# Attention, channel mix and gated convolution on one core: chunk 3's output moved ahead of the scores of chunk 5, two mixes moved up, and loads that wait for an earlier load to land

## The chip, the cores and the metric

The kernel runs on one core of a Trainium2 chip. The metric is the device time of one execution in microseconds. All times come from runs on the chip; the profile is one execution that the hardware profiler recorded.

## What is computed

The input has 2 sequences of 768 positions, 8 heads of 64 features each (512 features in all). Three stages follow one another:

```python
# 1. retention attention with decay lam per head, state kv_state carried along the sequence
intra = (q_b @ k_b.T * Dmask) @ v_b
inter = (q_b * lam_pow) @ kv_state
out[b] = intra + inter
kv_state = lam_block * kv_state + (k_b * rev_pow).T @ v_b
# 2. channel mix with a shift by one position, x = attention output
xk = mu_k * x + (1 - mu_k) * x_prev ; xr = mu_r * x + (1 - mu_r) * x_prev
x2 = sigmoid(xr @ w_r) * (relu(xk @ w_k) ** 2 @ w_v)
# 3. convolution gate of five taps, then projection
y = (sigmoid(conv(x2)) * (x2 @ w_val)) @ w_out
```

All arrays are float32. The reference walks stage 1 in blocks of 64 positions; the kernel uses chunks of 128, which gives the same sums.

## The kernel before

Stage 1 works in 12 chunks of 128 positions, chunks 0 to 5 of the first sequence and 6 to 11 of the second. The first chunk of a sequence has no inter part, the last has no state update. The order of each engine's work is written out by hand, and semaphores tie the engines together.

For a chunk n, **PE** does four things: `scores(n)` (L733, k times q into PSUM), `attend(n)` (L799, the weighted scores times v), `inter(n)` (L783, the state times the decayed q; this is the "state product" of the title) and `update(n)` (L761, decayed k times v). attend and inter add into the same two PSUM banks for a pair of chunks p = n // 2. Each is 8 matmuls in the code, 16 records in the profile. **DVE** weighs the scores with the decay (`weigh`, L508, two instructions of a chunk), makes the next state from the faded old one and the update (`new_state`, L525, L522 for the first of a sequence), and later the second half of the mix (`mix`, L532, four blocks of 128 features; tile xk_f), the low parts that the split products need (`mix_low`, L538, `low`, L543) and the 128x8 operation of L627. **ACT** fades the state (`fade`, L338, four instructions), copies the finished pair of chunks out of PSUM (`evacuate_x`, L330), makes the first half of the mix (`mix_part`, L355) and the high parts (`mix_high`, L361, `high`, L344). **POOL** decays k (`decay_k`, L286) and q (`decay_q`, L298).

What ties them around the change: scores(n) needs the weighing of chunk n - 2. weigh(n) needs scores(n). new_state(n) needs update(n) and the fade of the state before it. inter(n) needs the state of new_state(n - 1) and the decayed q. attend(n) needs the weighing of n. The first mix needs x of chunks 0 to 3, that is evacuate_x(1), which needs attend(3). `STATE_LAST` and `OUT_FIRST` tell which pairs have their inter last or first in the PSUM group.

Stage 2 begins with `hidden(0, 0)` in the middle of the last pair of chunks. It needs the low part of the mixed x (four mix_low) and of the first piece of w_k (`low`, piece 0). From there on PE works through products of 128x512 tiles in three passes each (L717 to L719).

All loads go out from **SP**, in the order in which they are needed: per chunk qk (512 KB) and kv (512 KB; 256 KB for chunks 0, 5 and 11, where k isn't needed), then w_k in four pieces, w_r in two, w_v in four. There are 8 buffers for chunks (`IN_BUFS`): a load of chunk 8 to 11 waits (`free`) until attend and update of the chunk eight before it are done; the others wait for nothing. The w_v loads wait for attend and update of chunk 7, since they lie on chunk buffers.

```python
def free(n):
    if n >= IN_BUFS:
        sp.wait_ge(att_done, n - IN_BUFS + 1)
        sp.wait_ge(update_done, updates(n - IN_BUFS))
```

Of the kernel before, what the change touches and what calls it, by code (L numbers as in the profile page):

```python
# [19 lines left out]
NCH = B * NCB  # L20
T = 512
NT = B * S // T
KT = DM // P
# [6 lines left out]
IN_BUFS = 8  # L30
# [4 lines left out]
CUTS = (0, 384, DM)  # L35
TURNED = 7
OUT_FIRST = 4


LAM_A, LAM_B, MU, CONV = 0, H, H + PAIRS, H + PAIRS + 2 * KT  # L40
# [12 lines left out]
def build(nc, prm_in, qk_in, v0_in, kv_in, w_k, w_v, w_r, w_val, w_out, out):  # L53
    with ExitStack() as ctx:
# [26 lines left out]
        wk_raw = place("wk_raw", [P, KT * DF], wk_at + 16 * KB)  # L81
# [127 lines left out]
        @block.sync  # L209
        def _(sp):  # L210
# [6 lines that stand above are left out]
            def load_qk(n):  # L217
                free(n)
                sp.dma_start(qk[n % IN_BUFS][:, :, :], qk_in[n]).then_inc(qk_here[n % IN_BUFS], 16)

            def load_kv(n):
                free(n)
                first = 0 if has_update(n) else 1
                sp.dma_start(kv[n % IN_BUFS][:, first:, :], kv_in[n, :, first:, :]).then_inc(kv_here[n % IN_BUFS], 16)

            def load_weight(raw, src, i, done):
                sp.dma_start(raw[:, i * PIECE:(i + 1) * PIECE], src[:, i * PIECE:(i + 1) * PIECE]).then_inc(done[i], 16)

            sp.dma_start(prm[:, :], prm_in).then_inc(prm_here, 16)
            load_qk(0)  # L230
            load_qk(1)
            sp.dma_start(kv[0][:, 1, :], v0_in).then_inc(kv_here[0], 16)
            load_qk(2)
            load_kv(1)
            load_qk(3)
            load_kv(2)
            load_qk(4)
            load_kv(3)
            load_qk(5)
            load_kv(4)  # L240
            load_kv(5)
            for p in range(3, NP - 1):
                load_qk(2 * p)
                load_qk(2 * p + 1)
                load_kv(2 * p)
                load_kv(2 * p + 1)
            load_qk(NCH - 2)
            load_qk(NCH - 1)
            load_weight(wk_raw, w_k, 0, wk_here)
            load_kv(NCH - 2)  # L250
            load_kv(NCH - 1)
            for i in range(1, 4):
                load_weight(wk_raw, w_k, i, wk_here)
            for i in range(2):
                load_weight(wr_raw, w_r, i, wr_here)
            sp.wait_ge(att_done, IN_BUFS)
            sp.wait_ge(update_done, updates(IN_BUFS - 1))
            for i in range(4):
                load_weight(wv_raw, w_v, i, wv_here)

            sp.wait_ge(h_done, FT * NT)
            for i in range(4):
                src = w_val if i < 2 else w_out
                sp.dma_start(w2_raw[:, i * PIECE:(i + 1) * PIECE],
                             src[:, i % 2 * PIECE:(i % 2 + 1) * PIECE]).then_inc(w2_here[i], 16)

            for n in range(OUT_CH):
                if n < OUT_CH - 1:
                    sp.wait_ge(out_ready, n + 1)
                    sp.dma_start(out[n * CH:(n + 1) * CH, :], out_sb[n // CT][:, n % CT, :]).then_inc(stored, 16)  # L270
                else:
                    for half in range(2):
                        cols = slice(CUTS[half], CUTS[half + 1])
                        sp.wait_ge(out_ready, n + 1 + half)
                        sp.dma_start(out[n * CH:(n + 1) * CH, cols], out_sb[n // CT][:, n % CT, cols]).then_inc(stored, 16)
            sp.wait_ge(stored, 16 * (OUT_CH + 1))
# [44 lines left out]
        def _(act):  # L321
            def evacuate_x(p):

                b, c = at(2 * p)
                cols = slice(b * SEG + HALO + c * CH, b * SEG + HALO + (c + 2) * CH)
                first = out_banks(2 * p)[0]
                act.wait_ge(att_done, 2 * p + 2)
                if p == OUT_FIRST:
                    act.wait_ge(inter_done, inters(2 * p + 1))
                nc.scalar.copy(x[:, :, cols].rearrange("p (g a) i -> p g a i", g=2),  # L330
                               ps[:, first:first + 2, :].rearrange("p g (a i) -> p g a i", a=2)).then_inc(x_ready, 1)

            def fade(n):

                act.wait_ge(state_ready, updates(n - 1))
                for a in range(PAIRS):
                    cols = slice(a * D, (a + 1) * D)
                    nc.scalar.activation(faded[:, cols], state[:, n % 4, cols], ACT.Copy,  # L338
                                         scale=qdec[:, a, CH - 1:CH]).then_inc(faded_ready, 1)
# [82 lines left out]
            fade(2)  # L422
            fade(3)
            evacuate_x(1)
            fade(4)
            for k in range(KT):
                mix_part(0, k, 0)
            evacuate_x(2)
            fade(7)
            for k in range(3):  # L430
                mix_high(0, k, 0)
            fade(8)
            evacuate_x(3)
            high(wk, wk_raw, 0, wk_here, wk_hi)
            fade(9)
            mix_high(0, 3, 0)
            high(wk, wk_raw, 1, wk_here, wk_hi)
            fade(10)
            for i in range(2, 4):
# [61 lines left out]
        def _(dve):  # L501
# [125 lines left out]
            nc.vector.tensor_scalar(om[:, :], prm[:, MU:MU + 2 * KT], -1.0, 1.0, ALU.mult, ALU.add).then_inc(om_ok, 1)  # L627
            dve.wait_ge(halo_ok, B)
            dve.wait_ge(om_ok, 1)
            for p in range(2, NP):  # L630
                new_state(2 * p)
                if p + 1 < NP:
                    weigh(2 * p + 2)
                    weigh(2 * p + 3)
                new_state(2 * p + 1)
                if p == 2:
                    mix(0, 0, 0)
                    mix(0, 1, 0)
                    mix(0, 2, 0)
                if p == 3:  # L640
                    mix(0, 3, 0)
                    mix_low(0, 0, 0)
                    mix_low(0, 1, 0)
                    mix_low(0, 2, 0)
                if p == 4:
                    mix_low(0, 3, 0)
                    low(wk, wk_raw, 0, wk_hi, wk_lo)
            for i in range(1, 4):
                low(wk, wk_raw, i, wk_hi, wk_lo)
# [63 lines left out]
        def _(pe):  # L713
# [56 lines left out]
            def inter(n):  # L770
                b, c = at(n)
                if c == 0:
                    return
                pe.wait_ge(qd_ready, inters(n))
                pe.wait_ge(state_ready, updates(n - 1))
                if opens(n, True):
                    if n < NCH - 2:
                        pe.wait_ge(x_ready, n // 2)
                    else:
                        pe.wait_ge(p_ready, 2 * n + 2)  # L780
                for a in (0, 2, 1, 3):
                    for row in range(2):
                        last = nc.tensor.matmul(place_of(n, row, a), state[rows_of(row), n % 4, a * D:(a + 1) * D],  # L783
                                                qd[rows_of(row), n % 4, a * P:(a + 1) * P],
                                                start=(opens(n, True) and a % 2 == 0),
                                                stop=(n == 2 * OUT_FIRST + 1 and a % 2 == 1), skip_group_check=True)
                last.then_inc(inter_done, 1)

            def attend(n):
                b, c = at(n)  # L790
                i = n % IN_BUFS
                pe.wait_ge(kv_here[i], 16 * (n // IN_BUFS + 1))
                pe.wait_ge(p_ready, 2 * n + 2)
                if n == 2 * OUT_FIRST:
                    pe.wait_ge(x_ready, OUT_FIRST)
                for a in range(PAIRS):
                    for row in range(2):
                        h = head_of(row, a)
                        last = nc.tensor.matmul(place_of(n, row, a), kv[i][:, 1, h * D:(h + 1) * D],  # L799
                                                pT[:, n % 4, row, a * P:(a + 1) * P],  # L800
                                                start=(opens(n, False) and a % 2 == 0),
                                                stop=(a % 2 == 1 and n % 2 == 1 and n // 2 != OUT_FIRST),
                                                skip_group_check=True)
                last.then_inc(att_done, 1)

# [94 lines left out]
            attend(2)  # L900
            scores(4)
            update(2)
            scores(5)
            update(3)
            inter(3)
            attend(3)
            update(4)
            for p in range(2, NP):
                if p + 1 < NP:
                    scores(2 * p + 2)  # L910
                    scores(2 * p + 3)
                if p == OUT_FIRST:
                    attend(2 * p)
# [86 lines left out]
```

## Time and profile before

| | us |
|---|---|
| median of 3 runs | 276.83 |
| lowest and highest | 275.75, 277.29 |
| the profiled execution | 276.0 |
| its span | 274.2 |
| PE busy | 269.9 |
| DVE busy | 166.0 |
| ACT busy | 125.4 |
| POOL busy | 23.6 |

The granted TensorE clock was 1.00 of full speed over the whole span. The span runs from the first to the last instruction; times in the views count from its start. In a timeline a row gives the start, the time from start to end of the merged instructions, engine and line, the operation, its tiles, the number of records and, in brackets, how long the engine stood idle before it and what ended that. Rows of neighbouring instructions overlap a little, since an instruction's end lies behind the next one's start. So what an instruction costs its engine is the distance from its start to the next one's start.

### The profile page before, as it was taken

The page shows a single profiled execution, that of the slowest core. Times are in us where ns is not written, and L with a number is a line of the kernel's source. Part 1 is how long each engine was busy: PE and PEld are TensorE (multiplying, and loading weights), DVE is VectorE, ACT ScalarE, POOL GpSimd, SP SyncE. Part 2 cuts the span into 40 slices and gives each one's busy share as a digit, 9 for nine tenths or more (in the row PEclk, how much of TensorE's full clock was granted, in tenths as well). Part 3 has the DMA queues.
Part 4 walks back from the last instruction along what each step waited for, and adds up shares of the span by engine and source line. Part 5 has one row for each costly group of instructions (what it writes and reads, how often), then busy time and mean ns, then how long its engine had stood idle before and what let it go on. Part 6 is the DMA issues. An engine that isn't in the chain of part 4 may idle for free.

```text
span 274.2 us, 4270 instructions
## 1 busy us (share of the span) xinstructions
PE 269.9 (98%) x1746; PEld 226.3 (83%) x1746; DVE 166.0 (61%) x258; ACT 125.4 (46%) x223; POOL 23.6 (9%) x25
## 2 busy tenths in 40 slices
PE   8999999999999999999999999999999999999996
PEld 7889977888888888888888888888888888888886
DVE  5866999998581125465885553429969599325000
ACT  2237788977582124365721234748217306412121
POOL 1667750000000000000000000000000000000000
PEclk9999999999999999999999999999999999999999
DMA  7999996000000000000000000530000000310323
GB/s 215 408 410 406 406 407 253 0 0 2 0 0 0 2 0 0 0 2 0 0 0 2 2 0 0 174 134 0 0 0 2 0 0 0 117 38 0 115 82 111
DMA packets 7506, 22.57 MB, mean 82 GB/s; under 512 B 960, under 2 KB 1216, under 8 KB 7488
## 3 DMA queue, kind: packets, MB, share of 16 engines
q1 hardware_dynamic: 7488, 22.31, 21.4%
q8 instruction: 14, 0.23, 0.3%
q14 instruction: 4, 0.03, 0.0%
HBM read 19.16 MB, written 3.15 MB: 81 GB/s over the span
## 4 chain that ended last, share of the span: by engine, by line
PE 96%; DVE 2%; DMA 1%; issue 0%; ACT 0%
PE ps L717 28%; PE ps L719 28%; PE ps L718 28%; PE ps L799 4%; PE ps L733 4%; PE ps L783 2%; PE ps L761 2%; DMA prm<-in_prm 1%; DVE dec L608 1%; DVE pT L508 0%; DVE qdec L589 0%; ACT out_sb L414 0%
## 5 line engine op out<-in xcount | busy, mean ns | idle before, releaser
L717 PE MATMUL ps<-xk_h,wk_h 128*128 128x512 f32 x96 | 37.5, 391 | 0.0
L718 PE MATMUL ps<-xk_l,wk_h 128*128 128x512 f32 x96 | 37.4, 389 | 0.0
L719 PE MATMUL ps<-xk_h,wk_l 128*128 128x512 f32 x96 | 37.4, 389 | 0.0
L717 PE MATMUL ps<-kk_h,wv_h 128*128 128x512 f32 x96 | 37.3, 389 | 0.0
L718 PE MATMUL ps<-kk_l,wv_h 128*128 128x512 f32 x96 | 37.3, 389 | 0.0
L719 PE MATMUL ps<-kk_h,wv_l 128*128 128x512 f32 x96 | 37.3, 389 | 0.0
L571 DVE SCALAR_TENSOR_TENSOR gate<-x,prm,gate 128x512 f32<-128x512 f32 x48 | 32.6, 748 | 0.0
L547 DVE SCALAR_TENSOR_TENSOR kk_f<-ps,ring 128x512 f32<-128x512 f32 x24 | 16.6, 691 | 24.1 <-ACT ring L367 24.1
L384 ACT ACTIVATE gate<-x,prm 128x512 f32<-128x512 f32 x12 | 8.7, 725 | 43.2 <-DVE x L557 43.2
L367 ACT ACTIVATE ring<-ps 128x512 f32<-128x512 f32 x24 | 14.3, 597 | 26.7 <-PE ps L719 26.7
L717 PEld LDWEIGHTS ps<-xk_h,wk_h 128*128 128x128 f32 x96 | 18.0, 188 | 4.0 <-issue 0.3
L719 PEld LDWEIGHTS ps<-xk_h,wk_l 128*128 128x128 f32 x96 | 18.0, 188 | 3.8
L718 PEld LDWEIGHTS ps<-kk_l,wv_h 128*128 128x128 f32 x96 | 18.0, 188 | 3.8
L719 PEld LDWEIGHTS ps<-kk_h,wv_l 128*128 128x128 f32 x96 | 18.0, 188 | 3.8
L557 DVE TENSOR_TENSOR x<-ps,r 128x512 f32<-128x512 f32 x12 | 8.3, 690 | 21.1 <-PE ps L719 21.1
L718 PEld LDWEIGHTS ps<-xk_l,wk_h 128*128 128x128 f32 x96 | 18.0, 188 | 3.7
L717 PEld LDWEIGHTS ps<-kk_h,wv_h 128*128 128x128 f32 x96 | 18.0, 188 | 3.7
L719 PE MATMUL ps<-w_h,gl 128*128 128x512 f32 (+2 forms) x52 | 19.6, 376 | 0.0
L718 PE MATMUL ps<-w_l,gh 128*128 128x512 f32 (+2 forms) x52 | 19.6, 376 | 0.0
L717 PE MATMUL ps<-w_h,gh 128*128 128x512 f32 (+2 forms) x52 | 19.5, 375 | 0.0
L717 PE MATMUL ps<-xr_h,wr_h 128*128 128x512 f32 x48 | 18.7, 389 | 0.0
L718 PE MATMUL ps<-xr_l,wr_h 128*128 128x512 f32 x48 | 18.7, 389 | 0.0
(74 smaller groups left out, 487.5 us busy)
## 6 DMA issues: line engine op xcount, KB each, us to landing
qk<-in_qk SPq DMA_DIRECT2D x12, 512.0 KB, 11.3
kv<-in_kv SPq DMA_DIRECT2D x9, 512.0 KB, 12.8
out<-out_sb SPq DMA_DIRECT2D x11, 256.0 KB, 2.0
wk_raw<-in_w_k SPq DMA_DIRECT2D x4, 512.0 KB, 14.2
wv_raw<-in_w_v SPq DMA_DIRECT2D x4, 512.0 KB, 12.5
wr_raw<-in_w_r SPq DMA_DIRECT2D x2, 512.0 KB, 15.0
w_raw<-in_w_val SPq DMA_DIRECT2D x2, 512.0 KB, 4.4
w_raw<-in_w_out SPq DMA_DIRECT2D x2, 512.0 KB, 6.9
```

The costliest lines, as they stand in the source:

```text
L367: nc.scalar.activation(ring[:, n % 4, :], ps[:, bank_of("mlp", t, n), :], ACT.Relu).then_inc(relu_ready, 1)
L384: nc.scalar.activation(like(t, gate[t][:, k, :]), x_cols(t, k, HALO), ACT.Copy, scale=prm[:, col:col + 1]).then_inc(tap0, 1)
L547: nc.vector.scalar_tensor_tensor(out=kk_f[:, n, :], in0=ps[:, bank_of("mlp", t, n), :], scalar=0.0, in1=ring[:, n % 4, :], op0=ALU.max, op ...
L557: nc.vector.tensor_tensor(x_cols(t, m, 1), like(t, ps[:, bank_of("mlp", t, FT + KT + m), :]), like(t, r[:, m, :]), ALU.mult).then_inc(x2_r ...
L571: nc.vector.scalar_tensor_tensor(out=like(t, gate[t][:, k, :]), in0=x_cols(t, k, HALO - j), scalar=prm[:, col:col + 1], in1=like(t, gate[t ...
L717: nc.tensor.matmul(to, left(0), right(0), start=(i == 0), stop=False)
L718: nc.tensor.matmul(to, left(0), right(1), start=False, stop=False)
L719: done = nc.tensor.matmul(to, left(1), right(0), start=False, stop=(i == last))
L733: last = nc.tensor.matmul(ps_s[n % 2][row][:, cols], qk[i][rows_of(row), 1, cols], qk[i][rows_of(row), 0, cols], start=True, stop=True)
L761: last = nc.tensor.matmul(ps[rows_of(row), ps_u[n % 2], a * D:(a + 1) * D], kdec[:, n % 4, at_k:at_k + D], kv[i][:, 1, h * D:(h + 1) * D], ...
L783: last = nc.tensor.matmul(place_of(n, row, a), state[rows_of(row), n % 4, a * D:(a + 1) * D], qd[rows_of(row), n % 4, a * P:(a + 1) * P], ...
L799: last = nc.tensor.matmul(place_of(n, row, a), kv[i][:, 1, h * D:(h + 1) * D], pT[:, n % 4, row, a * P:(a + 1) * P], start=(opens(n, False ...
```

## The change

On PE, attend(3) and inter(3) go ahead of scores(5), attend first, and update(4) goes between scores(6) and scores(7). For pair 1 the inter part is now the last to add into PSUM, so evacuate_x(1) waits for inter(3) too. On ACT two mix_parts go ahead of fade(4), and mix_high(3) goes up. On DVE mixes 0 and 1 go ahead of new_state(4), mix 3 ahead of the fourth pair's work, mix_low 3 beside the other three. On SP every load from the fifth on waits until an earlier load has landed.

```diff
+STATE_LAST = (1, OUT_FIRST)
...
+            def qk_landed(n):
+
+                sp.wait_ge(qk_here[n % IN_BUFS], 16 * (n // IN_BUFS + 1))
...
             load_qk(2)
+            qk_landed(0)
             load_kv(1)
+            qk_landed(1)
             load_qk(3)
+            kv_landed(0)
             load_kv(2)
+            qk_landed(2)
             load_qk(4)
+            kv_landed(1)
             load_kv(3)
...
             for p in range(3, NP - 1):
+                qk_landed(2 * p - 1)
                 load_qk(2 * p)
+                kv_landed(2 * p - 2)
                 load_qk(2 * p + 1)
+                kv_landed(2 * p - 1)
                 load_kv(2 * p)
+                qk_landed(2 * p)
                 load_kv(2 * p + 1)
+            qk_landed(NCH - 3)
             load_qk(NCH - 2)
+            kv_landed(NCH - 4)
             load_qk(NCH - 1)
+            kv_landed(NCH - 3)
             load_weight(wk_raw, w_k, 0, wk_here)
+            qk_landed(NCH - 2)
             load_kv(NCH - 2)
+            qk_landed(NCH - 1)
             load_kv(NCH - 1)
-            for i in range(1, 4):
-                load_weight(wk_raw, w_k, i, wk_here)
-            for i in range(2):
-                load_weight(wr_raw, w_r, i, wr_here)
+            sp.wait_ge(wk_here[0], 16)
+            load_weight(wk_raw, w_k, 1, wk_here)
+            kv_landed(NCH - 2)
+            load_weight(wk_raw, w_k, 2, wk_here)
+            kv_landed(NCH - 1)
+            load_weight(wk_raw, w_k, 3, wk_here)
+            sp.wait_ge(wk_here[1], 16)
+            load_weight(wr_raw, w_r, 0, wr_here)
+            sp.wait_ge(wk_here[2], 16)
+            load_weight(wr_raw, w_r, 1, wr_here)
...
-                if p == OUT_FIRST:
+                if p in STATE_LAST:
                     act.wait_ge(inter_done, inters(2 * p + 1))
...
             evacuate_x(1)
+            mix_part(0, 0, 0)
+            mix_part(0, 1, 0)
             fade(4)
-            for k in range(KT):
-                mix_part(0, k, 0)
+            mix_part(0, 2, 0)
+            mix_part(0, 3, 0)
             evacuate_x(2)
             fade(7)
-            for k in range(3):
+            for k in range(KT):
                 mix_high(0, k, 0)
...
-            mix_high(0, 3, 0)
...
             dve.wait_ge(om_ok, 1)
+            mix(0, 0, 0)
+            mix(0, 1, 0)
             for p in range(2, NP):
...
                 if p == 2:
-                    mix(0, 0, 0)
-                    mix(0, 1, 0)
                     mix(0, 2, 0)
+                    mix(0, 3, 0)
                 if p == 3:
-                    mix(0, 3, 0)
-                    mix_low(0, 0, 0)
-                    mix_low(0, 1, 0)
-                    mix_low(0, 2, 0)
+                    for k in range(KT):
+                        mix_low(0, k, 0)
                 if p == 4:
-                    mix_low(0, 3, 0)
                     low(wk, wk_raw, 0, wk_hi, wk_lo)
...
             update(2)
+            attend(3)
+            inter(3)
             scores(5)
             update(3)
-            inter(3)
-            attend(3)
-            update(4)
             for p in range(2, NP):
                 if p + 1 < NP:
                     scores(2 * p + 2)
+                    if p == 2:
+                        update(4)
                     scores(2 * p + 3)
```

The two edits of the stop flag in inter and attend follow `STATE_LAST` and are left out here.

PE, around chunks 3 to 7, before. qk_98 to qk_101 are the buffers of chunks 4 to 7, kv_104 to kv_106 those of chunks 2 to 4; L733 is scores, L761 update, L783 inter, L799 attend.

```order
L733 MATMUL ps<-qk_98 128x128 x8
L761 MATMUL ps<-kv_104,kdec 64x64 x8
L733 MATMUL ps<-qk_99 128x128 x8
L761 MATMUL ps<-kv_105,kdec 64x64 x8
L783 MATMUL ps<-qd,state 64x128 x8
L799 MATMUL ps<-pT,kv_105 64x128 x8
L761 MATMUL ps<-kv_106,kdec 64x64 x8
L733 MATMUL ps<-qk_100 128x128 x8
L733 MATMUL ps<-qk_101 128x128 x8
L783 MATMUL ps<-qd,state 64x128 x16
```

The same place now, where the lines of the file have moved: L764 is scores, L792 update, L814 inter, L830 attend.

```order
L764 MATMUL ps<-qk_98 128x128 x8
L792 MATMUL ps<-kv_104,kdec 64x64 x8
L830 MATMUL ps<-pT,kv_105 64x128 x8
L814 MATMUL ps<-qd,state 64x128 x8
L764 MATMUL ps<-qk_99 128x128 x8
L792 MATMUL ps<-kv_105,kdec 64x64 x8
L764 MATMUL ps<-qk_100 128x128 x8
L792 MATMUL ps<-kv_106,kdec 64x64 x8
L764 MATMUL ps<-qk_101 128x128 x8
L814 MATMUL ps<-qd,state 64x128 x16
```

attend(3) and inter(3) moved from behind update(3) to before scores(5), and update(4) moved into the pair of scores(6) and scores(7).

DVE, from the weighing of chunks 3 and 4 on, before. L508 weighs, L525 and L522 make a state, L532 mixes, L538 makes the low part of the mixed x.

```order
L508 TENSOR_TENSOR pT<-ps,dec 128x512 x4
L525 TENSOR_TENSOR state<-faded,ps 128x256
L508 TENSOR_TENSOR pT<-ps,dec 128x512 x2
L525 TENSOR_TENSOR state<-faded,ps 128x256
L627 TENSOR_SCALAR om<-prm 128x8
L525 TENSOR_TENSOR state<-faded,ps 128x256
L508 TENSOR_TENSOR pT<-ps,dec 128x512 x4
L532 SCALAR_TENSOR_TENSOR xk_f<-x,om,xk_f 128x512 x3
L522 COPY state<-ps 128x256
```

The same place now (L541 weighs, L558 and L555 make a state, L565 mixes).

```order
L541 TENSOR_TENSOR pT<-ps,dec 128x512 x4
L558 TENSOR_TENSOR state<-faded,ps 128x256
L541 TENSOR_TENSOR pT<-ps,dec 128x512 x2
L558 TENSOR_TENSOR state<-faded,ps 128x256
L660 TENSOR_SCALAR om<-prm 128x8
L565 SCALAR_TENSOR_TENSOR xk_f<-x,om,xk_f 128x512 x2
L558 TENSOR_TENSOR state<-faded,ps 128x256
L541 TENSOR_TENSOR pT<-ps,dec 128x512 x4
L565 SCALAR_TENSOR_TENSOR xk_f<-x,om,xk_f 128x512 x2
L555 COPY state<-ps 128x256
```

Two of the mixes moved in between the 128x8 operation and new_state(4), which is the third state update of these rows.

## Rows read from the trace of the kernel before

**Rows 1.** The page: span, PE's busy time, GB/s in 40 slices of 6.9 us.
```profile
span 274.2 us, 4270 instructions
...
PE 269.9 (98%) x1746; PEld 226.3 (83%) x1746; DVE 166.0 (61%) x258; ACT 125.4 (46%) x223; POOL 23.6 (9%) x25
...
GB/s 215 408 410 406 406 407 253 0 0 2 0 0 0 2 0 0 0 2 0 0 0 2 2 0 0 174 134 0 0 0 2 0 0 0 117 38 0 115 82 111
```

**Rows 2.** Timeline of PE, 34 to 41 us: attend(8) and the first hidden tile.
```profile
34.63 0.66 PE L799 MATMUL ps<-pT,kv 128*64 128x128 f32 x8
35.89 1.53 PE L799 MATMUL ps<-pT,kv 128*64 128x128 f32 x24 [0.61 <-issue]
...
40.65 0.47 PE L717 MATMUL ps<-xk_h,wk_h 128*128 128x512 f32 x1
```

**Rows 3.** Timeline of DVE, 35 to 42 us: low part of w_k's first piece.
```profile
39.30 1.21 DVE L543 TENSOR_TENSOR wk_l<-wk_raw,wk_h 128x1024 fp32r<-128x1024 f32 x1
```

**Rows 4.** Timeline of PE, 16 to 24 us: update(2) to inter(4) and inter(5).
```profile
16.98 0.69 PE L761 MATMUL ps<-kv,kdec 128*64 128x64 f32 x16
17.59 1.16 PE L733 MATMUL ps<-qk 64*128 64x128 f32 x16
18.68 0.69 PE L761 MATMUL ps<-kv,kdec 128*64 128x64 f32 x16
19.30 0.67 PE L783 MATMUL ps<-qd,state 64*64 64x128 f32 x16
19.89 1.09 PE L799 MATMUL ps<-pT,kv 128*64 128x128 f32 x16
20.82 0.64 PE L761 MATMUL ps<-kv,kdec 128*64 128x64 f32 x16
21.38 2.06 PE L733 MATMUL ps<-qk 64*128 64x128 f32 x32
23.37 1.10 PE L783 MATMUL ps<-qd,state 64*64 64x128 f32 x32
```

**Rows 5.** Instruction packets: all (page), 0 to 33.4 us, 33.4 to 33.6 us.
```profile
q8 instruction: 14, 0.23, 0.3%
...
q8 instruction: 3, 0.05, 0.6%
...
q8 instruction: 1, 0.02, 34.3%
```

**Rows 6.** Busy times by stretch: stretch, length, then busy us (instructions) of each engine.
```profile
0.00:33.40 33.40, 31.99 (x562) 29.00 (x564) 24.77 (x50) 15.32 (x37) 19.26 (x22) 1.00 0.96 368
...
0.00:208.00 208.00, 205.98 (x1456) 172.90 (x1457) 136.67 (x213) 104.88 (x188) 23.55 (x25) 1.00 0.25 93
0.00:236.70 236.70, 234.68 (x1583) 196.65 (x1584) 160.87 (x250) 117.50 (x209) 23.55 (x25) 1.00 0.22 84
```

**Rows 7.** Timelines of POOL and ACT: decay of q 3, evacuate_x(1).
```profile
17.18 1.28 POOL L298 TENSOR_TENSOR qd<-qk,qdec 128x512 f32<-128x512 f32 x1
...
21.04 1.02 ACT L330 COPY x<-ps 128x1024 f32<-128x1024 f32 x1 [1.23 <-PE ps L799]
```

**Rows 8.** Timeline of DVE, 18 to 29 us: states, the 128x8 operation, weighings, mixes.
```profile
18.30 0.41 DVE L525 TENSOR_TENSOR state<-faded,ps 128x256 f32<-128x256 f32 x1
...
20.33 0.70 DVE L627 TENSOR_SCALAR om<-prm 128x8 f32<-128x8 f32 x1
23.14 0.42 DVE L525 TENSOR_TENSOR state<-faded,ps 128x256 f32<-128x256 f32 x1 [2.12 <-ACT faded L338]
23.48 2.48 DVE L508 TENSOR_TENSOR pT<-ps,dec 128x512 f32<-128x512 f32 x4
25.88 2.77 DVE L532 SCALAR_TENSOR_TENSOR xk_f<-x,om,xk_f 128x512 f32<-128x512 f32 x3
```

**Rows 9.** Data packets from 0 to 33.4 us; loads of qk from issue to landing.
```profile
q1 hardware_dynamic: 3682, 12.24, 95.2%
...
DMA to landing us min/median/max: 3.9/11.3/15.7
```

More of the change, by code:

```diff
@@ L227, in load_weight, with kv_landed @@
                 sp.dma_start(raw[:, i * PIECE:(i + 1) * PIECE], src[:, i * PIECE:(i + 1) * PIECE]).then_inc(done[i], 16)
+            def qk_landed(n):
+                sp.wait_ge(qk_here[n % IN_BUFS], 16 * (n // IN_BUFS + 1))
+            def kv_landed(n):
+                sp.wait_ge(kv_here[n % IN_BUFS], 16 * (n // IN_BUFS + 1))
             sp.dma_start(prm[:, :], prm_in).then_inc(prm_here, 16)
@@ L233, in _ @@
             load_qk(2)
+            qk_landed(0)
             load_kv(1)
+            qk_landed(1)
             load_qk(3)
+            kv_landed(0)
             load_kv(2)
+            qk_landed(2)
             load_qk(4)
+            kv_landed(1)
             load_kv(3)
+            qk_landed(3)
             load_qk(5)
+            kv_landed(2)
             load_kv(4)
+            qk_landed(4)
             load_kv(5)
             for p in range(3, NP - 1):
+                qk_landed(2 * p - 1)
                 load_qk(2 * p)
+                kv_landed(2 * p - 2)
                 load_qk(2 * p + 1)
+                kv_landed(2 * p - 1)
                 load_kv(2 * p)
+                qk_landed(2 * p)
                 load_kv(2 * p + 1)
+            qk_landed(NCH - 3)
             load_qk(NCH - 2)
+            kv_landed(NCH - 4)
             load_qk(NCH - 1)
+            kv_landed(NCH - 3)
             load_weight(wk_raw, w_k, 0, wk_here)
+            qk_landed(NCH - 2)
             load_kv(NCH - 2)
+            qk_landed(NCH - 1)
             load_kv(NCH - 1)
-            for i in range(1, 4):
-                load_weight(wk_raw, w_k, i, wk_here)
-            for i in range(2):
-                load_weight(wr_raw, w_r, i, wr_here)
+            sp.wait_ge(wk_here[0], 16)
[8 more added lines that the diff above has]
+            load_weight(wr_raw, w_r, 1, wr_here)
             sp.wait_ge(att_done, IN_BUFS)
@@ L785, in inter @@
                                                 start=(opens(n, True) and a % 2 == 0),
-                                                stop=(n == 2 * OUT_FIRST + 1 and a % 2 == 1), skip_group_check=True)
+                                                stop=(a % 2 == 1 and n % 2 == 1 and n // 2 in STATE_LAST), skip_group_check=True)
                 last.then_inc(inter_done, 1)
@@ L801, in attend @@
                                                 start=(opens(n, False) and a % 2 == 0),
-                                                stop=(a % 2 == 1 and n % 2 == 1 and n // 2 != OUT_FIRST),
+                                                stop=(a % 2 == 1 and n % 2 == 1 and n // 2 not in STATE_LAST),
                                                 skip_group_check=True)
```

## Prediction

> **What bounds the kernel now.** I read the page first, then the timelines of PE, DVE, ACT and POOL over the attention stage, and last the DMA packets by queue and the busy times by stretch. The span is 274.2 us and the profiled execution took 276.0 us, so 1.8 us lie around the span; the median of the runs is 276.83 us, 0.83 above the profiled one, and they spread over 1.5 us. [Rows 1] show DMA near 408 GB/s from the second slice to the sixth and almost nothing after: all loads of chunks and of the first weights are one block that ends near 47 us. PE is the engine that runs through: 269.9 us busy. Between 9 us and the end its timeline has one bracket of idle time, 0.61 us for "issue" [rows 2], so whatever the change gains must come out of that, unless ordinary executions stand still more than this one.
>
> From the first hidden tile on (40.65 us, [rows 2]) PE never waits. So the change is worth what it does to the start of that tile, and the sum is made there. That tile needs two things: PE must have got through attention, and DVE must have made the low part of the first piece of w_k. [Rows 3] show that subtraction at 39.30 for 1.21, thus ending at 40.51, 0.14 before the tile starts. PE and DVE arrive together. This matters for the stall of [rows 2]: attend(8) breaks off after 8 of its 16 records, at 34.63, and goes on at 35.89, 1.26 us later. A whole attend takes 0.93 [rows 4], half of one 0.46, so the stall is 0.8; the 0.61 that the view counts as idle is its lower bound. Without it PE would be there at 39.85 and wait for DVE until 40.6. **Removing the stall alone buys 0.1 us at most.**
>
> **The stall itself.** It lies in the middle of one attend, where no semaphore is waited for. Its likely owner is in [rows 5]: a queue of instruction packets, 14 of them with 0.23 MB, 16 KB each, while PE has 2 x 1746 instructions, 249 for each packet. [Rows 6] let one count: between the packets near 208.0 and 236.7 us, when no loads run, PE's two columns rise by (1583 - 1456) + (1584 - 1457) = 254 instructions. The packet near 208.0 is the twelfth (two follow), and three had come by 33.4 [rows 5]. Stepping back eight from 1456 + 1457 = 2913 gives 881 for the fourth, but at 33.4, when that packet starts, 1126 are through. Under the load it came about 245 instructions late; at 1126 instructions in 33.4 us that is an estimated 5 to 7 us, and it starts 2.5 us before PE resumes. So I read the stall as a fetch behind queued loads.
>
> The Trainium skill, "Runtime: NRT & Kernel Launch", section on instruction fetch mechanics, speaks against this: PE's buffer holds 2048 instructions and a fetch is mostly hidden, so one that is 245 late would cost nothing. "DMA: Bandwidth & Descriptors", section on queues and rings, says that a DMA engine alternates between its queues packet by packet, so a deeper load queue should not delay another queue's packet. By these pages shallower loads remove nothing; the sum would be the first rival's.
>
> **Part 1, PE's order.** Costs from start to next start in [rows 4]: update after scores 0.61, scores after update 1.10, inter 0.59, attend 0.93, and scores(6) with scores(7) 1.99, so the second costs 0.89. From update(2) at 16.98 to inter(4) at 23.37 are 6.39 us. In the new order: update(2) 0.61, attend(3) 0.93, inter(3) 0.59, scores(5) 1.10, update(3) 0.61, scores(6) 1.10, update(4) 0.61, scores(7) 1.10 = 6.65. The same instructions in more alternation: **0.26 us more**.
>
> Two waits come with it. inter(3) is reached at 16.98 + 0.61 + 0.93 = 18.52. Its query is there (POOL, 17.18 + 1.28 = 18.46, [rows 7]), its state is not: DVE writes it at 18.30 for 0.41 [rows 8], and with 0.1 for the signal it is 18.8. **0.3 us of waiting.** Then scores(5) 19.4, update(3) 20.5, scores(6) 21.1, update(4) 22.2, scores(7) 22.8, inter(4) 23.9, and inter(5) is reached at 24.5.
>
> What does inter(5) need? The state that new_state(4) writes. With the same 0.1 DVE starts to weigh chunk 5 at 20.6, behind scores(5); the four weighings of [rows 8] take 2.48, so its two 1.2, to 21.8. The state update (0.41, overlapping its neighbour) brings it to 22.15, the 128x8 operation (0.70, likewise) to 22.75, and now the two moved mixes, 2.77 / 3 = 0.92 each, to 24.6. new_state(4) ends at 25.0, visible at 25.1: **0.6 us of waiting.** In the kernel before it started at 23.14 after 2.1 us of idleness; that idleness moves to 18.7 to 20.6, where DVE waits for scores(5), and the mixes fall behind it. Their input is no limit: ACT's evacuation (1.02) stood at 21.04 [rows 7], now attend(3) and inter(3) are done at 19.4 and x is there at 20.6, 2 us before DVE asks for the two parts that follow; the fade of state 4 can start at 22.3, and DVE wants it at 24.6.
>
> PE is then 0.26 + 0.3 + 0.6 = 1.15 us late, less rounding 1.1. I bound the two waits together by 0 and 1.2.
>
> **Part 2, the throttle.** Up to four loads, from qk 6 on three, are outstanding, and each new one waits for a landing. At 408 GB/s a 512 KB load takes 1.28 us. The quickest load from issue to landing took 3.9 us [rows 9], and 0.1 for SP to see a landing makes 4.0 for three loads, 1.33 each against 1.28. Over the ten throttled loads from qk 6 to qk 11 that is 0.5 us. By 33.4 us 12.24 MB had moved [rows 9]; qk 11 is the 22nd load, 11.0 MB in, so it was in at about 30.4 plus 1 to 2 us, and scores(11) will ask near 34.7. The slack of 2.5 us covers it. Behind SP's waits stand only further loads: w_v is last, and the value tiles that need it follow eight hidden and four receptance tiles. Where the half load kv 11 leaves less in flight, w_k's second piece may come 1 us later; hidden(0, 2) needs it, two tiles after the first. Cost on PE: 0.
>
> Gain: the fetch has at most three loads ahead, 3.8 us, instead of an estimated 5 to 7. It was missing 0.8, so the stall goes. **-0.8.**
>
> **Part 3, ACT and DVE.** The mixes go into DVE's chain earlier, so the end of that chain moves: in the kernel before 23.14 to 40.51 are 17.37 us of nearly unbroken work, now it starts at 24.6 and has two mixes fewer: 24.6 + 17.37 - 1.8 = 40.2, with small gaps 40.4. It is no longer what the first hidden tile waits for.
>
> **Sum:** 40.65 + 1.1 - 0.8 = 40.95, past DVE's 40.4. +0.3 us: span 274.5, time 276.3. That is against the profiled execution; against the median it reads as 0.5 us less, and either is within what a measurement can tell here (0.5%, about 1.4 us).
>
> **Rivals.**
> - *The stall stays* (the fetch does not care how deep the loads are queued, or it was no fetch). For: the three fetches before it left no gap. Against: it is late only under load [rows 6]. The two pages say the same as this rival. Time: 276.3 + 0.8 = 277.1. Chance 0.18.
> - *The throttle starves PE.* One mechanism: under load a landing is seen later than on a quiet queue, so three outstanding loads don't fill the engines. It decides once the pace passes 1.28 + 2.5 / 10 = 1.53 us per load, that is once issue to landing takes over 4.5 us with three outstanding. At 1.75 qk 11 lands 2.2 us late, and scores(11) and everything behind follow: 276.3 + 2.2 = 278.5 or, with kdec also late, 279.5: slower. For: the least value, 3.9, is no less than three loads' 3.84. Against: the slack. Chance 0.12.
> - *The waits don't form and the fetch cost more in ordinary executions.* If both state waits are 0, PE could be at 40.1 and DVE's 40.4 decides: -0.15, 275.8. If the 0.83 between the profiled execution and the median was a second stall that the throttle also removes, the new median is still 275.8 or, by the lowest run (275.75) less the same, down to 275.3. Chance 0.20.
> - *My forecast*, 276.3: 0.50.
>
> **Numbers.** Range 275.3 to 278.2: from the last rival's floor to just under the starved case, of which it leaves most out. Faster by over 0.5% (under 275.4) needs the third rival in full: 0.12. Slower by over 0.5% (over 278.2) is the starved case: 0.12. Same: 0.76.
>
> **What would show it.** Right: no "issue" gap on PE in attend(8); PE waits for DVE's state before inter(3) (0.3) and inter(5) (0.6); DVE idle about 2 us before the weighing of chunk 5 and not before new_state(4); DMA still near 400 GB/s up to 40 us; the first hidden tile at 40.9. Wrong: waits of PE for qk or kv, GB/s under 350, the issue gap still there, or inter(5) without a wait.

## The result and the profile after

The changed kernel took 281.5 us in the median of six runs (280.65 to 282.89), against 276.76 for the kernel before. That is 4.7 us slower, where I had forecast 276.3 and a range that ended at 278.2. The ratio, which is one of means, is 1.018 (interval 1.015 to 1.022), or 5.1 us; in the experiments the figures in brackets behind a ratio are its interval too. The profiled execution took 280.65 us, its span is 278.9.

From the first hidden tile to the end of the span both kernels take 233.6 us (274.2 - 40.65 before, 278.9 - 45.26 after). As foreseen, everything is in the start of that tile; it came 4.6 us later instead of 0.3.

The page of the changed kernel: the DMA share in tenths and the GB/s of 40 slices of 7.0 us, then two of its DMA issues with the median from issue to landing.

```profile
span 278.9 us, 4271 instructions
...
DMA  6989888800000000000000000250000000300223
GB/s 233 387 313 321 312 289 290 309 10 2 0 0 0 0 2 0 0 0 2 0 0 0 5 0 0 83 220 0 0 0 2 0 0 0 115 38 0 113 78 113
...
qk<-in_qk SPq DMA_DIRECT2D x12, 512.0 KB, 5.1
kv<-in_kv SPq DMA_DIRECT2D x9, 512.0 KB, 5.4
```

Against [rows 1] the load block has lost a quarter of its rate, from 408 to around 310 GB/s, and ends near 56 us instead of 47. This is the starved rival, and more of it than I had priced.

The waits of PE between 5 and 60 us (engine, line, tile, what it waited for: total, times, longest):

```profile
PE ps L764 <- DMA qk<-in_qk: 2.1, 2, 1.0
PE ps L814 <- POOL qd L330: 1.8, 2, 1.5
PE ps L792 <- issue: 0.4, 1, 0.4
```

In the kernel before, neither of the first two kinds stood behind scores(0). The timeline of PE from update(2) on, which answers to [rows 2, 4]:

```profile
16.69 0.69 PE L792 MATMUL ps<-kv,kdec 128*64 128x64 f32 x16
17.20 1.05 PE L830 MATMUL ps<-pT,kv 128*64 128x128 f32 x16
18.62 0.67 PE L814 MATMUL ps<-qd,state 64*64 64x128 f32 x16 [0.37 <-POOL qd L330]
19.22 1.16 PE L764 MATMUL ps<-qk 64*128 64x128 f32 x16
20.31 0.69 PE L792 MATMUL ps<-kv,kdec 128*64 128x64 f32 x16
20.92 1.16 PE L764 MATMUL ps<-qk 64*128 64x128 f32 x16
22.02 0.69 PE L792 MATMUL ps<-kv,kdec 128*64 128x64 f32 x16
23.74 1.16 PE L764 MATMUL ps<-qk 64*128 64x128 f32 x16 [1.03 <-DMA qk<-in_qk]
24.83 1.10 PE L814 MATMUL ps<-qd,state 64*64 64x128 f32 x32
...
36.04 2.40 PE L764 MATMUL ps<-qk 64*128 64x128 f32 x32 [1.02 <-DMA qk<-in_qk]
38.37 1.97 PE L830 MATMUL ps<-pT,kv 128*64 128x128 f32 x32
...
43.64 0.67 PE L814 MATMUL ps<-qd,state 64*64 64x128 f32 x16 [1.47 <-POOL qd L330]
44.23 1.09 PE L830 MATMUL ps<-pT,kv 128*64 128x128 f32 x16
45.26 0.50 PE L748 MATMUL ps<-xk_h,wk_h 128*128 128x512 f32 x1
```

Four things are to be seen. scores(7) waits 1.0 us for its load, scores(10) waits 1.0 us for qk 10, and inter(10) waits 1.5 us for its decayed q. attend(8), at 38.37, runs through without the gap of [rows 2]. And inter(5), the second half of the row at 24.83, does not wait: the wait for qk has given DVE the time to make its state. The "issue" gap of 0.4 us, before update(9) at 34.33, is most likely a late load as well: POOL waits for kv 9 and ends its decay at 34.23 (below), 0.1 us before PE goes on. Counted from start to next start, all these waits cost PE about 5.5 us; less the gap of 0.8 us that is gone, that is the 4.8 us by which the way from attend(0) to the first hidden tile has grown (37.1 us against 32.3).

Why is the decayed q late? The timeline of POOL:

```profile
32.67 1.56 POOL L318 TENSOR_TENSOR kdec<-kv,dec 128x512 f32<-128x512 f32 x1 [0.54 <-DMA kv<-in_kv]
...
40.32 1.06 POOL L318 TENSOR_TENSOR kdec<-kv,dec 128x512 f32<-128x512 f32 x1 [2.74 <-DMA kv<-in_kv]
41.34 3.48 POOL L330 TENSOR_TENSOR qd<-qk,qdec 128x512 f32<-128x512 f32 x2
```

POOL decays k of chunk 10 before q of chunk 10, and so q, whose load was in since 36 us, stands behind the load of kv 10, for which POOL waits 2.7 us. I had not followed that queue. By the landings in the trace qk 10 and qk 11 came at 36.0 and 37.2 us, in the kernel before at 30.9 and 32.2: 5 us later, while kv 5, the last load ahead of qk 6, came at 19.3 or 19.4 in both.

Where do the engines stand still? The busy times by stretch of the changed kernel, half a microsecond each; the last three numbers are PEclk, the busy share of the 16 DMA engines and GB/s:

```profile
16.50:17.00 0.50, 0.50 (x16) 0.38 (x14) 0.19 (x1) 0.00 (x0) 0.50 (x1) 1.00 0.95 369
17.00:17.50 0.50, 0.50 (x20) 0.50 (x16) 0.50 (x2) 0.00 (x0) 0.50 (x2) 1.00 0.88 340
17.50:18.00 0.50, 0.50 (x14) 0.50 (x10) 0.50 (x1) 0.00 (x0) 0.50 (x1) 1.00 0.43 152
18.00:18.50 0.50, 0.25 (x6) 0.01 (x1) 0.42 (x2) 0.04 (x1) 0.50 (x1) 1.00 0.20 45
18.50:19.00 0.50, 0.38 (x13) 0.38 (x16) 0.00 (x0) 0.50 (x3) 0.26 (x2) 1.00 0.57 135
19.00:19.50 0.50, 0.50 (x16) 0.33 (x10) 0.00 (x0) 0.50 (x4) 0.50 (x1) 1.00 0.97 369
```

qk 5 landed at 17.50, and SP issued qk 6 at 17.51. But at that moment the engines had almost finished kv 4 and kv 5, which were to bridge the time: the share falls to 0.2 and is back only at 19.0, 1.5 us after the issue. The completions that the trace has for each of the 16 engines tell why. For qk 5 fifteen engines had reported between 15.67 and 16.50; the last reported at 17.50. A landing is the slowest of 16, and this one trailed by a microsecond. When SP sees it, the others have used up that much of what is queued behind. A single engine does not trail so far every time: over the ten loads from qk 6 to qk 11 the first and the last report lie 1.8 us apart in the median (0.5 to 2.6). For the quickest load, the first of the kernel before, they lie 0.5 us apart.

### The profile page after: what moved, and what is told of

Its sections match the earlier page's. It is cut to its first block, busy times and chain, and to the rows that moved or that the text cites. A ratio compares the mean times of both kernels' runs of the same rounds, so it can differ in the third digit from the quotient of the medians.

```text
span 278.9 us, 4271 instructions
## 1 busy us (share of the span) xinstructions
PE 271.3 (97%) x1746; PEld 227.0 (81%) x1746; DVE 168.8 (61%) x258; ACT 125.8 (45%) x223; POOL 25.3 (9%) x25
## 4 chain that ended last, share of the span: by engine, by line
PE 86%; POOL 6%; issue 5%; POOLq 1%; DVE 1%; ACT 0%
PE ps L748 28%; PE ps L749 27%; PE ps L750 27%; POOL qd L330 4%; POOL kdec L318 2%; PE ps L919 1%; POOLq L55 1%; PE ps L830 1%; PE ps L764 1%; DVE pT L541 0%; PE ps L814 0%; DVE qdec L622 0%; DVE kdec L628 0%; ACT out_sb L446 0%; POOLq L329 0%
```

## The experiments

The first experiments separate the two halves of the change and take the throttle deeper. In the runs by depth all loads up to w_r are issued by one list, and load i waits for load i - DEPTH:

```diff
+            for i, (z, n) in enumerate(loads):
+                if i >= DEPTH:
+                    landed(*loads[i - DEPTH])
```

**The order alone.** The changed kernel with SP's stream of the kernel before:

```diff
             load_qk(2)
-            qk_landed(0)
             load_kv(1)
-            qk_landed(1)
             load_qk(3)
```

and so on for all landing waits.

> The changed order on PE, ACT and DVE, with the loads issued as in the kernel before. Theory 1 (the throttle starves the DMA engines and that is the whole loss): loads at about 405 GB/s again, no wait of PE for qk or qd beyond 0.4 us, the order itself costs 0.3 to 1 us: 277.0 to 277.8 us. Theory 2 (the new order costs the time through PE's waits for state and for decayed q, which the late loads only accompany): 279 us or more.

It took 277.63 us (12 runs, 275.54 to 278.86), ratio 1.0036 (1.0013 to 1.0060); 409 GB/s between 20 and 40 us. Theory 1 held. Of the loss the order has 0.9 us by medians, 1.0 by the ratio. But the timeline of PE in this execution holds more gaps for "issue" than the kernel before had:

```profile
24.76 1.16 PE L783 MATMUL ps<-qd,state 64*64 64x128 f32 x32 [0.63 <-issue]
...
31.82 0.49 PE L733 MATMUL ps<-qk 64*128 64x128 f32 x4 [1.31 <-issue]
...
38.72 1.53 PE L799 MATMUL ps<-pT,kv 128*64 128x128 f32 x24 [0.41 <-issue]
```

**The throttle alone.** The kernel before with the landing waits of the change:

```diff
             load_qk(2)
+            qk_landed(0)
             load_kv(1)
+            qk_landed(1)
             load_qk(3)
```

> The order of the kernel before, with the throttle. Theory 1: the loads come at about 300 GB/s, the last chunk loads and the decayed q of chunk 10 are as late as in the changed kernel, and the first hidden tile starts near 45 us: 280.5 to 282 us. Theory 2: below 278 us.

281.86 us (5 runs), ratio 1.020 (1.018 to 1.022), 297 GB/s between 20 and 40 us. Theory 1 held: the throttle by itself makes the whole loss, and the order, which costs 1.0 alone, costs nothing to be seen beside it. That its waits fall where PE waits for loads anyway would explain that; for inter(5) the timeline above shows it.

**Depth four in the changed order.**

> The changed kernel, but every load up to w_r waits for the landing of the fourth load ahead of it (the change has that up to kv 5, and the third from qk 6 on). Theory 1a (a landing is the slowest of 16 engines, 1 to 1.7 us behind the others, and new data flows 1.4 us after the issue, so about 3 us of data must still be queued at a landing): three loads of 1.28 us are 3.84 us, enough; only the half loads leave short gaps: rate 380 GB/s or more, 276.5 to 278 us. Theory 1b (the lag of the slowest engine keeps growing): rate 330 to 350 GB/s, 278.5 to 280 us.

278.08 us (6 runs), ratio 1.0064 (1.0047 to 1.0081), between the two: the rate of 1b (338 GB/s), but nearly the time of 1a. PE waited 0.9 us for qk and 1.2 us for decayed q. No "issue" gap. So my figure of 3 us that must be queued was too small.

**Depth six in the changed order.**

> As the last, with the sixth load ahead. Theory 1a: full rate, the issue gap of attend(8) may come back in part: 276.5 to 277.5 us, within 0.5 us of the run with the order alone. Theory 1b: the same rate as with the order alone. If the issue gap is a fetch that waits behind queued loads, it is shorter than 0.8 us here; if not, it is as with the order alone.

277.68 us (6 runs), ratio 1.0054 (1.0035 to 1.0073), 407 GB/s. Full rate, as foreseen, and the time of the order alone; the gap of attend(8) is there in full, so six deep is as deep as no throttle for whatever makes it. This run shows the order's own waits without late loads; the timeline of PE:

```profile
18.84 0.67 PE L782 MATMUL ps<-qd,state 64*64 64x128 f32 x16 [0.32 <-DVE state L526]
...
23.94 0.67 PE L782 MATMUL ps<-qd,state 64*64 64x128 f32 x16
25.12 0.67 PE L782 MATMUL ps<-qd,state 64*64 64x128 f32 x16 [0.52 <-DVE state L526]
...
37.19 1.53 PE L798 MATMUL ps<-pT,kv 128*64 128x128 f32 x24 [0.58 <-issue]
```

inter(3) waits 0.32 and inter(5) 0.52 for DVE's state. The stretch of DVE that makes inter(5) wait, from the weighing of chunk 5 to new_state(4):

```profile
20.64 1.29 DVE L509 TENSOR_TENSOR pT<-ps,dec 128x512 f32<-128x512 f32 x2 [1.96 <-PE ps L732]
21.85 0.41 DVE L526 TENSOR_TENSOR state<-faded,ps 128x256 f32<-128x256 f32 x1
22.18 0.16 DVE L628 TENSOR_SCALAR om<-prm 128x8 f32<-128x8 f32 x1
22.43 2.22 DVE L533 SCALAR_TENSOR_TENSOR xk_f<-x,om,xk_f 128x512 f32<-128x512 f32 x2
24.57 0.41 DVE L526 TENSOR_TENSOR state<-faded,ps 128x256 f32<-128x256 f32 x1
```

The next experiments look for a version that beats both.

**Depth five in the order of the kernel before**, the list as above with 5.

> The kernel before with nothing changed but its loads: each waits for the landing of the fifth load ahead. Theory: four loads left at a landing are 5.1 us of data, enough for full rate (400 GB/s or more) in every order, so the starvation is gone: within 0.5 us of the kernel before. If depth also sets how late instructions are fetched, the 0.6 us issue gap of attend(8) is gone or shorter; since DVE is as late as PE at the first hidden tile, that gains 0.2 us at most in an execution like the profiled one. Rival (a throttle costs in itself, by SP's waits between issues): 277.5 us or more.

276.11 us (12 runs), ratio 0.9977 (0.9960 to 0.9993), 406 GB/s. The starvation is gone, and this is the fastest kernel of the study, 0.6 us ahead of the kernel before. The reason I gave is not shown: in the profiled execution the gap of attend(8) stands, at 0.56 us.

**The fade first**, loads as before:

```diff
-            evacuate_x(1)
             fade(4)
+            evacuate_x(1)
```

> The kernel before with ACT's fade of state 4 ahead of the evacuation of pair 1, loads as before. DVE's wait of 2.1 us before new_state(4) shrinks to about 0.6, its chain ends 1.5 us earlier, and the first hidden tile no longer waits for it. Theory (fetch gaps on PE are what remains): 276.0 to 276.8 us, PE with its issue gaps still sets the start. Rival (DVE's chain was the bound in most executions): 275.0 to 275.8 us.

276.97 us (12 runs, of which one took 1541.9 us and is not in the ratio), ratio 1.0006 (0.9986 to 1.0025): no difference. DVE's wait shrank to 1.2 us, and in the profiled execution its low part was ready at 41.3, 1.6 us before the first hidden tile. That fits the theory; DVE's chain alone was not the bound. The profiled execution held four "issue" gaps on PE, 0.2 to 0.8 us.

**Both together.**

> The last two together. Theory (issue gaps are late fetches, and depth sets the lateness): no issue gap in attention and the first hidden tile at 39.9 to 40.1 us: 275.5 to 276.1 us, with less spread. Rival (five loads deep is as deep as six for the fetch): the gap of 0.6 us stays and the time is that of the kernel with the fade moved alone.

276.21 us (12 runs), ratio 0.9982 (0.9967 to 0.9996). Of the rival one half held: the gaps stay (0.8, 0.5 and 0.4 us in the profiled execution). The other half, the time of the kernel with the fade moved alone (276.97), did not: it is the time of depth five alone (276.11), to which the moved fade adds nothing.

**The mixes back, depth six in the changed order.**

```diff
-            mix(0, 0, 0)
-            mix(0, 1, 0)
             for p in range(2, NP):
...
                 if p == 2:
-                    mix(0, 2, 0)
-                    mix(0, 3, 0)
+                    for k in range(KT):
+                        mix(0, k, 0)
```

with ACT's two mix_parts back behind fade(4).

> The changed kernel at depth six, with the two mixes back behind the weighing of chunks 6 and 7 (ACT's two halves of them behind the fade of state 4). Theory (the mixes ahead of new_state(4) made inter(5) wait for its state): inter(5)'s wait of 0.5 us for DVE is gone or under 0.2, the wait of inter(3) of 0.3 stays, and the time is 0.3 to 0.5 us less than with the mixes moved at depth six (277.7): 277.2 to 277.4 us. Rival: DVE's chain now ends later than PE arrives, and nothing is gained.

277.73 us (12 runs), ratio 1.0038 (1.0021 to 1.0055). PE's waits hold none for DVE's state any more, and DVE writes the state for inter(5) at 23.25 instead of 24.57, so the cause of inter(5)'s wait is shown; but the time is that of depth six. In the profiled execution inter(3) waited 0.85 us for its decayed q instead, and three issue gaps add up to 1.7 us. A wait of half a microsecond taken away is not to be seen under these.

The last experiments test how the rate goes with depth, and whether update(4) matters.

**Depth two in the changed order.**

> The changed kernel with every load waiting for the landing of the second one ahead. Theory (time from issue to landing over depth sets the pace; at depth three the chunk loads came 1.7 us apart, 5.1 us over three): a load alone took 3.9 us, with some lag of the slowest engine 4.0 to 4.4, over two 2.0 to 2.2 us per load, 240 to 260 GB/s; qk 11 lands about 7 us later than in the changed kernel: 286 to 290 us. Rival (the rate is capped near 300 GB/s by something that comes with the throttle but not with its depth): 281 to 282 us.

296.55 us (4 runs), ratio 1.073 (1.069 to 1.077); 228 GB/s between 20 and 40 us. The direction and the mechanism held, the size did not: a load of 524 KB at 228 GB/s is 2.3 us, not 2.0 to 2.2, and PE's late work added to it. PE waited up to 3.9 us at a stretch, and the mean granted clock of 20 to 40 us fell to 0.83, so TensorE ran at times at the lower of its two levels, 1.2 GHz instead of 2.4. The scores right behind the wait of 3.9 us took 2.08 us instead of 1.16. The last three numbers are again the clock, the DMA share and GB/s:

```profile
20.00:40.00 20.00, 14.79 (x245) 13.12 (x242) 13.15 (x18) 8.12 (x20) 10.03 (x8) 0.83 0.72 228
```

**Depth four in the order of the kernel before.**

> The order of the kernel before at depth four. In the changed order depth four gave 333 GB/s, fetches 3.4 to 3.7 us late and no issue gap. Theory: the same here, the gap of attend(8) gone, but the decayed q of chunk 10 comes late and PE waits 1 to 1.5 us for it or for qk: 277.0 to 278.0 us, slower than at depth five. Rival (freedom from late fetches outweighs the slower loads): 275.5 to 276.3 us.

278.98 us (6 runs), ratio 1.0086 (1.0058 to 1.0114), 342 GB/s. The theory's direction held, but it is 1 us slower than expected: besides 1.5 us for qk and 0.5 for decayed q, the first hidden tile waited for w_k's low part. Not its load was late: ACT had made the high part by 38.2 us. DVE came to the low part only at 41.20 and took 2.29 us over it, where it took 1.21 in the kernel before [rows 3]; why it took so long was not tested.

```profile
PE ps L732 <- DMA qk<-in_qk: 1.5, 3, 0.8
PE ps L716 <- DVE wk_l L542: 1.2, 1, 1.2
PE ps L760 <- issue: 0.6, 1, 0.6
PE ps L782 <- POOL qd L297: 0.5, 1, 0.5
```

At full rate the changed order is 1.0 us slower than the old one. At depth four it is faster by medians (278.08 against 278.98), by 0.6 us if each is set against the kernel before in its own series, and there the intervals overlap (1.0047 to 1.0081, 1.0058 to 1.0114). It has scores(5) behind attend(3) and inter(3) and so asks for its load later, which would explain a difference, but none is shown.

**update(4) back ahead of scores(6)**, the changed order without the throttle:

```diff
             update(3)
+            update(4)
             for p in range(2, NP):
                 if p + 1 < NP:
                     scores(2 * p + 2)
-                    if p == 2:
-                        update(4)
                     scores(2 * p + 3)
```

> The order of the change without the throttle, but update(4) back ahead of scores(6). Theory (the order costs by PE's change-overs and two waits for state): scores(6) and scores(7) adjoin again, which saves 0.1 us of change-over, the waits stay: within 0.3 us of the run with the order alone (277.6 us). Rival (update(4) between the scores is what holds up DVE and PE): 276.5 to 277.0 us.

277.89 us (12 runs), ratio 1.0026 (0.9998 to 1.0053), as with the order alone: the place of update(4) makes no difference that can be seen.

The rate between 20 and 40 us by depth, changed order and order before:

| depth | changed order: GB/s, us | order before: GB/s, us |
|---|---|---|
| 2 | 228, 296.55 | |
| 3 from qk 6 on (the change) | 306, 281.50 | 297, 281.86 |
| 4 | 338, 278.08 | 342, 278.98 |
| 5 | | 406, 276.11 |
| 6 | 407, 277.68 | |
| none | 409, 277.63 | 407, 276.8 |

## Why the prediction was wrong

**The step that failed** is in part 2: "The quickest load from issue to landing took 3.9 us, and 0.1 for SP to see a landing makes 4.0 for three loads, 1.33 each against 1.28." That is the time of the first load of all, on quiet engines. In the changed kernel loads took 5.1 (qk) and 5.4 us (kv) in the median, 1.7 and 1.8 for each of three outstanding, and the ten loads from qk 6 to qk 11 landed 1.8 us apart (19.4 to 37.2 us), beyond the 1.53 at which my own rival said it decides. The term of 0.5 us for these ten loads was in truth 5. Two things were missing. A landing is reported by the last of 16 engines, under load 1.8 us behind the first in the median; in the first load that lag was 0.5 us, so the 3.9 of [rows 9] holds little of it. And kv 5 is only half a load: with it outstanding 1.9 us of data are queued, not 2.6. After the engines had run dry at 18 us the rate stayed low, at 289 to 321 GB/s in slices of 7 us. That depth decides is shown by the depths: the rate rises with each step from 228 to 406 GB/s and is full at five. That it is the lag of the slowest engine that makes a load take 5 us or more is read from the reports of the engines, not tested.

**The starved rival** had the right mechanism and place, but its price of 2.2 us or, with kdec also late, 3.2, was too low, and its chance of 0.12 too. It counted the lateness of qk 11 alone, and put that at 2.2 us beyond its slack of 2.5; it landed 5 us later than before. The first late load was already one of pair 3 (1.0 us at scores(7)), where I had looked at no slack at all, and the last and largest wait, 1.5 us, came through POOL's queue, where q 10 stands behind kv 10.

**Part 1 held.** Computed 0.26 for change-overs, 0.3 and 0.6 for inter(3) and inter(5), 1.15 in all. At depth six the waits measured 0.32 and 0.52, and from attend(0) to the first hidden tile were 1.2 us more than in the kernel before (33.5 against 32.3), with the gap of attend(8) in both. The order alone cost 1.0 us (0.4 to 1.7). A little luck was in it: the 128x8 operation took 0.16 us instead of 0.70 and the two mixes 2.22 instead of 1.85, and the two errors nearly cancel. Taking the mixes back removed inter(5)'s wait. In the changed kernel itself it didn't form, because late loads stood in front of it. There inter(3) waited 0.37 us, but for POOL's decayed q.

**Part 3** held where the loads were on time: DVE's low part of w_k was ready at 40.34 us at depth six, computed 40.4, while PE came at 41.92. In the changed kernel it was ready at 42.5, still ahead of PE.

**The gap of attend(8) held too, as far as it is a fetch behind queued loads**, but not that a shallower queue would give it back for nothing. In three executions PE resumed 2.4 to 2.5 us after the start of the instruction packet concerned: at 33.4 and 35.89 in the kernel before [rows 2, 5], and so with the order alone and at depth six. The stretch of 0.2 us that holds that packet at depth six, and the busy times up to it:

```profile
q8 instruction: 1, 0.02, 34.5%
...
0.00:34.70 34.70, 32.81 (x562) 29.41 (x564) 26.36 (x53) 15.93 (x38) 20.11 (x23) 1.00 0.96 374
```

562 + 564 = 1126 instructions, exactly as in [rows 6], and PE resumes at 37.19. In the changed kernel the fourth packet starts at 31.7:

```profile
q8 instruction: 1, 0.02, 20.2%
...
0.00:31.70 31.70, 29.52 (x490) 26.24 (x492) 23.58 (x47) 12.89 (x31) 15.48 (x19) 1.00 0.87 316
```

982 instructions are through, not 1126: by the count of the prediction (881) it is 101 late instead of 245, and attend(8) has no gap. That is not only because PE itself was slower there: from the start of PE's instruction 881 to the start of the packet were 6.1 us in the kernel before and 2.9 in the changed one. (The prediction's estimate of 5 to 7 us was right, but its division, 245 instructions at 1126 in 33.4 us, gives 7.3.) All 13 profiles fall into two groups. In the eight with five or more loads outstanding or no limit the packet is 6.1 to 7.5 us late, and the gap stands at the same place, after 1181 instructions of PE. In the five of depth four and less it is 2.9 to 5.4 us late, and there is no gap at that place. The other "issue" gaps of over 0.2 us in the first group stand after 437, 685 or 933 instructions, 248 apart like the packets. So the gap of 0.8 us did go, as forecast, but it went with the loss: it needs a depth of four or less, while the full rate needs five. At this size of load no depth that was run gives both. Whether removing the stall alone would buy 0.1 us stays open, since no run at full rate was without it.

Of the two pages weighed there, "Runtime: NRT & Kernel Launch" in the Trainium skill, section on instruction fetch mechanics, lets PE hold 2048 instructions; here PE stood still when a packet came 245 instructions late, so this trace does not agree. "DMA: Bandwidth & Descriptors" in the Trainium skill, section on queues and rings, lets an engine alternate between its queues by packet. The lateness of 101 against 245 instructions by depth does not bear out that this keeps another queue's packet from waiting.

The rival with the cheaper fetches in ordinary executions (275.3 to 275.8) did not come about, and its floor of 275.3 does not follow from its own terms: 275.75 less 0.15 is 275.6. The sum of +0.3 us would have needed full rate at depth three.

What is still open: why depth five gains 0.6 us over no throttle in the old order. The profiled execution had no fewer gaps in attend(8). That SP's issues are spread out, or that fetches early in the program come sooner, was not told apart. Nor was the lag of the slowest engine tested by itself: an issue that hangs on the twelfth of 16 completions, which for qk 5 came 1.3 us before the last, would do it, and it was not tried. Nor is it known why one engine trails: in the changed kernel it does so by 0.9 to 1.1 us in the loads that land from 15.0 to 19.4 and from 36.0 to 38.5 us, each time after an instruction packet that took 0.9 to 1.0 us (12.1 and 31.7 us), but the packet of 26.2 us left no such mark.

## What to carry to other kernels

A throttle on loads must leave in flight, at the moment in which a landing is seen, the data for the time until newly issued loads keep the engines busy (here 1.5 us) plus the lag of the slowest engine behind the first (here 1.8 us in the median), so count the depth from loads under load and never from the fastest load on a quiet queue, and count half loads as halves. Before a stream is delayed, find the first consumer whose slack is gone and every engine's queue in which another's input stands behind the late one. Work that is moved ahead of a state update is free only while nobody waits for that state: here DVE's idle 2 us did not vanish, they moved.

## What the runs showed of the hardware beside this

**The start of the program varies.** The 16 records of scores(0) took 1.16 us in the kernel before, 1.67 in the changed one and 2.07 with the order alone, in a part of the program that is the same in all; the first two rows of PE after the warm-up in the run with the order alone:

```profile
4.88 2.07 PE L733 MATMUL ps<-qk 64*128 64x128 f32 x16
6.88 0.66 PE L742 MATMUL ps<-ident,qk 128*128 128x128 f32 x4
```

attend(0) began between 7.4 and 8.7 us over all profiles, so single executions are compared better from there: from attend(0) to the first hidden tile were 32.3 us in the kernel before, 37.1 in the changed one, 34.9 with the order alone, 33.5 at depth six. What decides it is not settled; the half pace would fit TensorE's lower clock level, but the profile gives 1.00 for that stretch.

**Late fetches go with the spread.** With the order alone single executions went from 275.54 to 278.86 us, and the profiled one, at 278.84, held 2.4 us of "issue" gaps. The profiled executions of the fade moved alone (278.27 us) and of update(4) moved back (278.28) held 2.1 and 2.3 us of them, that of the kernel before (276.0) 0.6. That they cause the whole spread is not shown. Such a stretch of short matmuls under full load traffic is where one execution is no measurement.
